# Two-MLP attention kernel: the high part of w1 comes by rounding transfers from POOL's queue, not by copies on ScalarE

## The reference

```python
scores = scale * np.matmul(q, k.transpose(0, 1, 3, 2))
cum = np.cumsum(np.maximum(s, 0.0), axis=-1)
bias = -(cum[:, :, :, None] - cum[:, :, None, :])
scores = np.where(causal, -1000000000.0, scores + np.minimum(bias, 0.0))
attn = softmax(scores)                     # rows, with 1e-9 added to the sum
x = attn @ v                               # 2304 x 512
h = np.maximum(np.maximum(x @ w1, x @ w2), x @ w3)      # 2304 x 768
y = h @ w_out                              # 2304 x 512
out = ((y @ w_a) * (y @ w_b)) @ w_out2     # 1536 wide inside
```

## Time and profile before

| | |
|---|---|
| median of three runs | 982.7 us |
| the profiled execution | 982.89 us |
| its span in the profile | 981.1 us |
| PE busy | 941.4 us (96%) |
| VectorE (DVE) busy | 465.4 us (47%) |
| ScalarE (ACT) busy | 406.4 us (41%) |
| POOL busy | 215.7 us (22%) |
| DMA, mean over the span | 60 GB/s |

### The profile page before, as it was taken

The page is one execution under the profiler, slowest core; times in us unless marked ns, Lnnn a source line. Parts: engine busy times, 40 slices in busy tenths (PEclk is TensorE's granted clock), DMA queues, the critical chain, the costliest instruction groups (busy, mean ns, idle before and its releaser), DMA issues.

```text
span 981.1 us, 15222 instructions
## 1 busy us (share of the span) xinstructions
PE 941.4 (96%) x5776; PEld 859.0 (88%) x5776; DVE 465.4 (47%) x1054; ACT 406.4 (41%) x912; POOL 215.7 (22%) x309
## 2 busy tenths in 40 slices
PE   3789899999999999999999999999999999999998
PEld 2588899999999999999999888888888888888898
DVE  6789788877666577563233433221122112211212
ACT  4778677676655556543223432211121112111211
POOL 6868554453432423410000000000000000000000
PEclk9999999999999999999999999999999999999999
DMA  3644322222121221100032332200020001000100
GB/s 115 225 147 141 96 85 71 68 75 77 63 79 39 84 65 53 48 2 27 16 130 88 101 97 92 77 9 1 0 82 5 1 1 65 1 0 1 43 1 22
DMA packets 29240, 58.74 MB, mean 60 GB/s; under 512 B 3184, under 2 KB 15568, under 8 KB 29136
## 3 DMA queue, kind: packets, MB, share of 16 engines
q1 hardware_dynamic: 29168, 57.77, 18.4%
HBM read 47.82 MB, written 9.88 MB: 59 GB/s over the span
## 4 chain that ended last, share of the span: by engine, by line
PE 93%; issue 2%; DVE 1%; DMA 1%; ACT 1%; POOL 1%; SPq 0%; DVEq 0%; POOLq 0%; ACTq 0%
PE bank L1175 30%; PE bank L1047 23%; PE bank L1190 15%; PE bank L1067 8%; PE bank L998 6%; PE bank L1028 6%; PE bank L1014 5%; DMA qk_st<-cum_row 1%; DVE soft L790 0%; DMA qk_raw<-in_qk 0%; POOL soft L486 0%; ACT soft L536 0%; SPq L383 0%; DMA x_raw<-in_s 0%; POOL qk_st L477 0%
## 5 line engine op out<-in xcount | busy, mean ns | idle before, releaser
L957 DVE TENSOR_TENSOR g_raw<-bank,a_sb 128x512 f32<-128x512 f32 (+1 forms) x60 | 38.3, 638 | 298.5 <-PE bank L1175 298.5
L1047 PE MATMUL bank<-xs_hi,w_hi 128*128 128x256 f32 (+1 forms) x576 | 174.0, 302 | 1.9 <-DVE xs_lo L811 1.2
L1047 PE MATMUL bank<-xs_hi,w_lo 128*128 128x256 f32 (+1 forms) x576 | 170.7, 296 | 0.0
L1047 PE MATMUL bank<-xs_lo,w_hi 128*128 128x256 f32 (+1 forms) x576 | 170.6, 296 | 0.0
L486 POOL TENSOR_SCALAR soft<-soft,rden 128x576 f32<-128x576 f32 (+4 forms) x160 | 102.1, 657 | 216.6 <-DVE rden L776 216.6
L1175 PE MATMUL bank<-y_hi,w2b_hi 128*128 128x512 f32 (+1 forms) x360 | 132.4, 368 | 0.0
L1175 PE MATMUL bank<-y_lo,w2b_hi 128*128 128x512 f32 (+1 forms) x360 | 132.4, 368 | 0.0
L1175 PE MATMUL bank<-y_hi,w2b_lo 128*128 128x512 f32 (+1 forms) x360 | 132.4, 368 | 0.0
L1047 PEld LDWEIGHTS bank<-xs_hi,w_hi 128*128 128x128 f32 x576 | 109.4, 190 | 3.4 <-DVE xs_lo L811 1.4
L702 ACT ACTIVATE a_sb<-bank 128x512 f32<-128x512 f32 (+1 forms) x60 | 33.3, 555 | 188.5 <-PE bank L1175 188.5
L536 ACT ACTIVATE soft<-soft,neg_max 64x576 f32<-64x576 f32 (+4 forms) x160 | 96.0, 600 | 35.4 <-DVE neg_max L790 34.2
(11 more groups left out here) (84 smaller groups left out, 1825.7 us busy)
## 6 DMA issues: line engine op xcount, KB each, us to landing
qk_raw<-in_qk SPq DMA_DIRECT2D x32, 576.0 KB, 3.8
w_raw<-in_w SPq DMA_DIRECT2D x40, 384.0 KB, 3.6
v_raw<-in_v SPq DMA_DIRECT2D x32, 160.0 KB, 2.2
y_raw<-y_dram SPq DMA_DIRECT2D x4, 1024.0 KB, 5.5
outT<-o_stage SPq DMA_DIRECT2D x16, 256.0 KB, 2.1
qk_raw<-in_qk SPq DMA_DIRECT2D x8, 256.0 KB, 3.2
y_dram<-m_tmp SPq DMA_DIRECT2D x8, 160.0 KB, 1.8
y_dram<-h_raw SPq DMA_DIRECT2D x8, 160.0 KB, 1.8
```

Of the source, the lines that this page charges most:

```text
L1047: ins = nc.tensor.matmul(up_ps[g][:, 0:width1(c)], up1_w(w, f, g, kc), x[:, kc, 0:width1(c)], start=(kc == 0 and at == 0), stop=(kc == KC ...
```

## The change

- ScalarE's sixteen copies `w1_hi_copy` are taken out, with their semaphore `w1_hi_done`.
- POOL issues eight transfers (`round_w1`), each of two pieces (128 x 1536), from the weights in DRAM straight into `w1_hi`. The source is fp32 and the destination float32r, so the transfer rounds. The first is issued between `upper(1)` and the two memsets ahead of slot 0, the others in slots 1 to 7 after the slot's normalisations.
- SP's loads into `w1_raw` stay, since the low parts need the original. The weights of the first MLP are thus read twice.
- Both subtractions that make `w1_lo` now wait for the load of their piece and for the transfer of their pair. Their own place in the order stays.

```diff
-        w1_hi_done, w1_lo_done, w1_rest_done = sem("w1_hi_done"), sem("w1_lo_done"), sem("w1_rest_done")
+        w1_rounded = [sem(f"w1_rounded{p}") for p in range(N_P1 // 2)]
+        w1_lo_done, w1_rest_done = sem("w1_lo_done"), sem("w1_rest_done")
...
             def w1_rest_sub(piece):
-                pool.wait_ge(w1_hi_done, piece + 1)
+                pool.wait_ge(w1_loaded[piece], 16)
+                pool.wait_ge(w1_rounded[piece // 2], 16)
...
+            def round_w1(pair):
+
+                cols = slice(2 * pair * PIECE, 2 * (pair + 1) * PIECE)
+                nc.gpsimd.dma_start(w1_hi[:, cols], w1[:, cols]).then_inc(w1_rounded[pair], 16)
+
             upper(0)
             upper(1)
+            round_w1(0)
...
                 for k in range(tile_count(n)):
                     normalise(n, k)
+                if 0 < n < N_P1 // 2:
+                    round_w1(n)
                 for piece in W1_PIECES.get(n, []):
                     w1_rest_sub(piece)
...
-            def w1_hi_copy(piece):
-                act.wait_ge(w1_loaded[piece], 16)
-                cols = slice(piece * PIECE, (piece + 1) * PIECE)
-                nc.scalar.activation(w1_hi[:, cols], w1_raw[:, cols], ACT.Copy).then_inc(w1_hi_done, 1)
...
-                for piece in W1_PIECES.get(n, []):
-                    w1_hi_copy(piece)
...
             def w1_lo_sub(piece):
-                dve.wait_ge(w1_hi_done, piece + 1)
+                dve.wait_ge(w1_loaded[piece], 16)
+                dve.wait_ge(w1_rounded[piece // 2], 16)
```

## The result

The changed kernel takes 989.38 us (median of four executions, 988.74 to 990.16), the kernel before beside it 982.75 us: a ratio of 1.0068, 95% interval 1.0056 to 1.0081. It is slower by 6.7 us (the ratio less one, times 982.7; the two medians differ by 6.6), beyond the 0.2% that the prediction took as the least that can be told from no change. The forecast was 986.3 us with a range of 982.6 to 993.0. The direction and the range held; the sum was 3.1 us short, and the likeliest case's own range of 984.5 to 988.5 missed it.

The account below looks back on a forecast made before the run. The prediction took POOL to pace the attention-alone stage, whose end shifts the PE-bound MLP one for one. From 982.9 us, +2.5 for POOL's issues, +1.0 for transfers and -0.15 for ScalarE's copies gave 986.3 us, range 982.6 to 993.0.

Parts of the forecast that it names:

- the likeliest case: Each issue holds POOL near 1.15 us, giving 986.3 us, own range 984.5 to 988.5; chance 0.55.
- The copies are worth nothing: ScalarE's sixteen copies: removing them gains only 0.15 us, in slot 8; the others were priced at nothing.
- The first two issues are free: POOL, ahead of slot 0 and in slot 1: both issues fall where POOL idles or waits anyway, at no cost.
- The waits of the low parts cost nothing: The w_lo subtractions: transfers land well before use, five or six slots later for pairs 1 to 7; cost nothing.
- Eight issues on POOL: POOL, slots 2 to 6: five issues of 1.15 us, less idle time and a PE wait, cost +2.5 us.
- T: Time one transfer issue holds POOL: taken as 1.15 us, with ends of 0.45 and 3.6 us.
- The rival that priced it so: Cheap issue on POOL, below 0.64 us: gaps hold all five, only part of DMA term left, 982.7 to 983.8 us; chance 0.20.
- The transfers themselves: DMA engines, 30 to 50 us: some 2 us do not fit, ahead of upper(9)'s q and k load; +1.0 us, between 0 and 2.
- The text's own sign for this error: Loads of q and k landing after 8 us would show that the DMA term was too small.
- Its signs of being right: Slot 7's normalisation and the MLP start 3 to 4 us later; POOL's idle gone in slots 3 to 7; gaps grown about 1.15 us.
- POOL paces slots 1 to 8: Attention-alone stage: POOL, with under half a microsecond to spare a slot, is the engine that paces it.
- The stalls behind VectorE: Rival: each issue on POOL also waits out a 1.0 us VectorE subtraction, giving 991.4 us; chance 0.20.

Follow-up runs that it names:

- issues alone: Kernel before, copies kept, plus eight tiny POOL transfers (128 x 16 values) into a spare buffer at the change's places: 983.44 us, ratio 1.0005.
- bytes alone: Kernel before, copies kept, plus eight plain fp32 transfers of 0.786 MB from ScalarE's queue into spare buffers, one a slot: 987.99 us, ratio 1.0051.
- the rows of 1 KB: Plain fp32 transfers from ScalarE's queue (987.99 us), same bytes in rows of 1 KB instead of 6 KB: 989.03 us, ratio 1.0064.
- one placement of the issue: Changed kernel with pairs 3 to 7 transferred in slots 8 to 12: issued behind the normalisations 991.46 us, issued ahead of them 985.70 us.

## Why the prediction was right in direction and short in size

*Right.* The kernel is slower. The end moves one for one with the start of the MLP: 6.0 us at 64.47, and both profiles in step from there but for the clock of one stretch. The copies are worth nothing (full transfers with the copies kept: the time of the change). The first two issues are free; the bytes of the first transfer are not quite, since POOL's `upper` of slot 1 starts at 17.69 us behind its q and k load, before and with issues alone at 16.92 and 16.94. The waits of the low parts cost nothing: in the view of the w_hi tile no engine idled ahead of a `w_lo` for a transfer.

*Eight issues on POOL: +2.5 us, the first step that failed.* T was taken at 1.15 us from POOL's own tensor instruction; it measured 0.61. By the prediction's own formula, 5T - 2.3 - 0.9, that is nothing, and issues alone measured +0.5 us (-0.4 to 1.4). This was the mechanism that carried most of the forecast, and it was not the cause. The nearer row was SP's 0.36 to 0.60 us for half the bytes, which had been taken for a bound. The rival that priced it so was right about the price and wrong about the time, since it left the DMA term at 1 us.

*The transfers themselves: +1.0 us, between 0 and 2; the step that decided.* This term measured 5.0 us (3.5 to 6.5) by bytes alone, and it is most of 6.7. The failing thought was the budget: demand against free engine time, on the mean of 30 to 50 us, with the overflow laid on a single load. In 20 to 30 us the engines had been 40% busy, with room for a transfer by that reckoning, and the chain lost 2.4 us there all the same, on a bias row of 4 KB. What a latency-bound chain pays is the queue that each of its loads meets, and it has several loads a slot: the bias rows and the q and k loads above all got later. The load that the prediction named, that of `upper(9)`, is among them, at 7.8 us instead of 4.9. The text's own sign for this error, q and k loads landing after 8 us, came: the longest took 9.3 us to land, before 6.0. Its signs of being right did not: slot 7 was 6.0 us late and not 3 to 4, and POOL's idle times had not gone but moved in front of loads.

*POOL paces slots 1 to 8: not borne out.* POOL was nearly full, but in the chain of before its pieces from 10 to 60 us come to 8.4 of 50 us, beside 9.3 of PE, 8.4 of DMA, 7.5 of ScalarE and 7.3 of VectorE: it is one link of a chain through all engines. With its work lightened, at ScalarE's expense, the stage did not shorten. Lateness of POOL does count in part: with issues alone, slot 7 was 2.0 us late, and the same execution ended 1.1 us later. A full engine whose every instruction ends just ahead of a wait looks like the pacer and need not be one.

The two errors had opposite signs (2.5 too much; 5.7 too little, if the whole rest of the 6.7 is put on the transfers), which is why the sum stood within 3.1 us. That it came so near, and that the range held, owes as much to luck as to the reading of the trace. The stalls behind VectorE, priced at a T of 2.15 us, did not come: of eight issues the longest took 0.743 us.

## What to carry to other kernels

Price a transfer that is added to a latency-bound stage by what each critical load behind it waits, up to its whole length (here 0.786 MB, 2.4 us; one row paid that, another 1.0), and not by the free share of the DMA engines: the same kind of transfer cost about 0.8 us each up to slot 7 (6.1 us over eight) and nothing in slots 8 to 12. Replacing work on an engine with slack by a second read of the same data won nothing here. Where two engines hold each other up, the place of a short instruction can matter more than its length: move it into a wait of its own engine.

## What was not expected of the hardware

- A 4 KB row can wait for most of a large transfer on another queue. On the chain it took 1.7 us before; issued 0.12 us after POOL began to issue 0.786 MB it took 4.13 and landed at 24.3 us, and the large transfer, 4.6 us after its own issue at 20.09, at 24.7. Two more kernels with that transfer from POOL have the row at 4.38 and 4.24 us. The Trainium skill's "DMA: Bandwidth & Descriptors", in "Queues, rings and completion order", has each DMA engine take turns between its queues by whole packets, typically of 9 to 17 descriptors. The profile counts 1152 pieces for POOL's eight transfers, nine for each transfer and engine; if such nine are one packet in that sense, the row waits for nearly a whole transfer, as the trace has it. Where such a packet ends no run here shows: the rows of 1 KB (987.99 and 989.03 us) were tried on ScalarE's queue, where the two rows on the chain took 2.38 and 3.32 us with the large pieces.
- Transfers that convert fp32 to float32r filled the engines as plain ones did: all traffic together, SP's loads included, ran at 332 GB/s against 333 in 40 to 50 us. No such transfer was timed by itself. From POOL they landed after 6.3 us in the median, the plain ones from ScalarE after 4.8 and 5.2 (two buffers), and whether the rounding, the queue or the place makes the difference is not shown.
- VectorE's subtraction of two SBUF tensors, 0.94 us beside a POOL instruction before, took 3.20 us when it began during an issue on POOL with three tensor instructions unbroken behind it. That POOL's run is the cause is a reading of these traces, in which it comes with one placement of the issue and goes with the other, and of the 5.8 us between the two; it was not measured by itself.
